# Windowed attention and two MLPs on one core: the first steps reordered, a gate in its own buffers, and an addition moved between engines

## The reference

```python
# q, k, v: (4, 8, 576, 64) float32; window 64
scores = (1/sqrt(64)) * q @ k.T                       # per batch and head
rel = pos[:, None] - pos[None, :]
scores = where((rel >= 0) & (rel < 64), scores, -1e9)
scores = scores - max(scores)
attn = exp(scores); attn = attn / (sum(attn) + 1e-09)
x = (attn @ v) as (2304 tokens, 512)
# first MLP: d_model 512, d_ff 1536
xn = x / sqrt(mean(x*x) + 1e-06) * rms_g
g = xn @ w_gate
x = (g * sigmoid(g) * (xn @ w_val)) @ w_out
# second MLP: d_ff 2048
h = x @ w_in
out = (h * sigmoid(1.702 * h)) @ w_out2
```

## Time and profile before

| | us |
|---|---|
| median of 3 runs | 904.75 |
| lowest and highest | 903.81 and 905.58 |
| the profiled execution, whole | 904.1 |
| its span, first to last instruction | 901.6 |
| TensorE busy, in the span | 889.1 |
| VectorE busy | 539.6 |
| ScalarE busy | 398.5 |
| POOL busy | 82.2 |
| mean granted TensorE clock | 0.998 of 2.4 GHz |

### The profile page before, as it was taken

The page is one execution under the profiler, slowest core; times in us unless marked ns, Lnnn a source line. Parts: engine busy times, 40 slices in busy tenths (PEclk is TensorE's granted clock), DMA queues, the critical chain, the costliest instruction groups (busy, mean ns, idle before and its releaser), DMA issues.

```text
span 901.6 us, 14706 instructions
## 1 busy us (share of the span) xinstructions
PE 889.1 (99%) x5372; PEld 771.3 (86%) x5372; DVE 539.6 (60%) x1256; ACT 398.5 (44%) x941; POOL 82.2 (9%) x114
## 2 busy tenths in 40 slices
PE   8899999999999999999999999999999999999998
PEld 7799888888888888888888899999999999999997
DVE  6886634334333343433336578887788788867663
ACT  5676333343333423334123354545464554545442
POOL 6234001030010300113000000000000000000000
PEclk9999999999999999999999999999999999999999
DMA  7672111102111021100500222121432122241201
GB/s 253 205 218 96 51 51 51 50 24 74 51 50 51 24 73 51 51 25 1 186 1 24 94 96 69 60 81 47 164 117 94 48 74 67 67 145 47 71 24 70
DMA packets 41078, 69.75 MB, mean 77 GB/s; under 512 B 3632, under 2 KB 13872, under 8 KB 41008
## 3 DMA queue, kind: packets, MB, share of 16 engines
q1 hardware_dynamic: 39600, 67.12, 23.0%
q10 hardware_dynamic: 1408, 1.70, 0.6%
HBM read 59.38 MB, written 9.44 MB: 76 GB/s over the span
## 4 chain that ended last, share of the span: by engine, by line
PE 94%; DVE 3%; ACT 2%; issue 1%; POOL 1%; POOLq 0%; ACTq 0%; DVEq 0%
PE ps L631 16%; PE ps L633 15%; PE ps L632 15%; PE ps L825 7%; PE ps L826 7%; PE ps L824 7%; PE ps L767 7%; PE ps L763 7%; PE ps L765 6%; PE ps L612 2%; PE ps L584 2%; PE ps L598 2%; DVE w_all L1197 1%; ACT prob L867 0%; DVE sig L1235 0%
## 5 line engine op out<-in xcount | busy, mean ns | idle before, releaser
L631 PE MATMUL ps<-x_hi,w_all 128*128 128x512 f32 (+1 forms) x480 | 179.4, 374 | 0.2 <-DVE x_lo L1137 0.2
L633 PE MATMUL ps<-x_lo,w_all 128*128 128x512 f32 (+1 forms) x480 | 176.7, 368 | 0.0
L632 PE MATMUL ps<-x_hi,w_all 128*128 128x512 f32 (+1 forms) x480 | 176.7, 368 | 0.0
L826 PE MATMUL ps<-w2out,hB 128*128 128x512 f32 x288 | 113.0, 392 | 0.0
L825 PE MATMUL ps<-w2out,hB 128*128 128x512 f32 x288 | 112.9, 392 | 0.0
L824 PE MATMUL ps<-w2out,hB 128*128 128x512 f32 x288 | 112.0, 389 | 0.0
L631 PEld LDWEIGHTS ps<-x_hi,w_all 128*128 128x128 f32 x480 | 90.4, 188 | 18.4 <-issue 3.0
L633 PEld LDWEIGHTS ps<-x_lo,w_all 128*128 128x128 f32 x480 | 90.4, 188 | 15.3
L632 PEld LDWEIGHTS ps<-x_hi,w_all 128*128 128x128 f32 x480 | 90.4, 188 | 14.6
L1235 DVE SCALAR_TENSOR_TENSOR sig<-sig,ps 128x512 f32<-128x512 f32 x48 | 32.9, 686 | 107.1 <-ACT sig L981 107.1
L631 PE MATMUL ps<-h_hi,w_all 128*128 128x512 f32 (+1 forms) x240 | 90.4, 376 | 1.8 <-DVE hid L1244 1.6
(11 more groups left out here) (144 smaller groups left out, 1557.0 us busy)
## 6 DMA issues: line engine op xcount, KB each, us to landing
wstage<-in_w_b SPq DMA_DIRECT2D x48, 512.0 KB, 3.7
wstage<-in_w_a SPq DMA_DIRECT2D x36, 256.0 KB, 3.2
vwin<-in_v_win SPq DMA_DIRECT2D x32, 256.0 KB, 3.9
kwin<-in_k_t SPq DMA_DIRECT2D x32, 160.0 KB, 3.3
x2raw<-x_scratch SPq DMA_DIRECT2D x3, 1536.0 KB, 7.5
out_dram<-yB SPq DMA_DIRECT2D x18, 256.0 KB, 4.4
qtok<-in_q_t SPq DMA_DIRECT2D x34, 128.0 KB, 2.6
x_scratch<-wstage SPq DMA_DIRECT2D x3, 1024.0 KB, 4.2
```

What stands on the lines that cost most here:

```text
L631: pe.matmul(out_, w[:, 0, cols], xh, start=first, stop=False, **flags)
L632: pe.matmul(out_, w[:, 1, cols], xh, start=False, stop=False, **flags)
L633: return pe.matmul(out_, w[:, 0, cols], xl, start=False, stop=last, **flags)
L826: ins = pe.matmul(y, hB_of(g, chunk, 1)[:, rows], w[:, 0, chunk, :], start=False, stop=last)
```

## The change

It has three parts. (1) In the first four steps the orders on all four engines are changed: the transposes of a step go ahead of the product with V of the step before, two groups of fillers go, ScalarE takes four of the first nine casts where it had one, in which (0, 1) is between the copies and (2, 1) behind `inverse_rms(0)`, and VectorE's splits follow a new order `FIRST_SPLITS`. That order also sets the numbers that SP's loads wait for. (2) In tile 0 the scaled gate of chunk 1 lies in `ss` and its tanh in `sq`, so that scaling and tanh of chunk 1 run directly behind those of chunk 0. (3) From step 4 on the 1e-9 is added to the sums by ScalarE, in an activation of 128x4 with a wait for its own exponentials, and VectorE makes only the reciprocal. Besides, the splits (4, 0) and (4, 1) of tile 0 stand behind the normalising of step 5, where (4, 0) was between those of steps 4 and 5.

```diff
+        def scaled_of(c):
+            return ss[:, GT:2 * GT] if c == 1 else gsc
+
+        def silu_of(t, c):
+            return sq[:, :] if (t, c) == (0, 1) else sig[:, 0:TILES_A[t][1]]
...
+        FIRST_SPLITS = ((0, 0), (0, 1), (1, 0), (1, 1), (2, 0), (0, 2), (2, 1), (1, 2), (2, 2))
+
         def splitsA(c, m):
-            return 3 * c + m + 1
+            return FIRST_SPLITS.index((c, m)) + 1 if c < 3 else 3 * c + m + 1
+
+        CASTS_BY_ACT = ((0, 1), (1, 1), (2, 0), (2, 1)) + tuple((c, m) for c in range(3, CA) for m in range(2))
+        CASTS_BY_POOL = ((0, 0), (1, 0), (0, 2), (1, 2)) + tuple((c, 2) for c in range(2, CA))
...
@@ gpsimd
             weights_hi_A(0, 0)
             normalise(1)
             normalise(2)
-            weights_hi_A(0, 1)
             normalise(3)
-            weights_hi_A(0, 2)
             weights_hi_A(1, 0)
             add_early_square(1)
-            weights_hi_A(1, 1)
-            weights_hi_A(1, 2)
+            weights_hi_A(0, 2)
             add_early_square(2)
             add_early_square(3)
-            weights_hi_A(2, 1)
+            weights_hi_A(1, 2)
             weights_hi_A(2, 2)
...
@@ tensor
             keep_busy(3, 2)
+            transpose_probs(2)
             probs_by_v(1)
-            transpose_probs(2)
+            transpose_probs(3)
             pe.wait_ge(max_ready, EARLY)
-            keep_busy(4, 2)
             probs_by_v(2)
-            transpose_probs(3)
-            first_chunk_part(0)
             probs_by_v(3)
-            for d in range(1, DC):
+            for d in range(DC):
                 first_chunk_part(d)
...
@@ scalar
                 ins.then_inc(exp_done, 1)
+                if s >= EARLY:
+                    act.wait_ge(exp_done, s + 1)
+                    act.wait_ge(consts_ready, 2)
+                    by = rsum[:, s % EARLY, :]
+                    nc.scalar.activation(by, by, ACT.Identity, bias=guard[:, 0:1]).then_inc(sums_guarded, 1)
...
             first_x_hi(0)
+            weights_hi_by_act(0, 1)
+            copy_probT(2)
             first_x_hi(1)
-            copy_probT(2)
-            first_square(0)
             copy_probT(3)
-            first_square(1)
             first_x_hi(2)
-            first_square(2)
             first_x_hi(3)
+            for s in range(EARLY):
+                first_square(s)
+            weights_hi_by_act(1, 1)
             nc.scalar.preload_act_table_set(LN_SET)
-            first_square(3)
             weights_hi_by_act(2, 0)
             act.wait_ge(consts_ready, 1)
             inverse_rms(0)
+            weights_hi_by_act(2, 1)
...
-                    tanh_A(t, c)
+                    if (t, c) != (0, 1):
+                        tanh_A(t, c)
+                    if (t, c) == (0, 0):
+                        tanh_A(0, 1)
...
@@ vector
             def reciprocal_of_sum(s):
+                if s >= EARLY:
+                    dve.wait_ge(sums_guarded, s - EARLY + 1)
+                    wait(dve, probs_normed, s - EARLY + 1)
+                    nc.vector.reciprocal(rrec[:, s % EARLY, :], rsum[:, s % EARLY, :]).then_inc(late_rec, 1)
+                    return
...
             weights_lo_A(0, 0)
+            reciprocal_of_sum(3)
             evacuate_probT(1)
-            reciprocal_of_sum(3)
             dve.wait_ge(g_loaded, 16)
             first_x_lo(0)
             weights_lo_A(0, 1)
             first_x_lo(1)
-            weights_lo_A(0, 2)
+            weights_lo_A(1, 0)
             first_x_lo(2)
-            weights_lo_A(1, 0)
             first_x_lo(3)
             weights_lo_A(1, 1)
+            weights_lo_A(2, 0)
+            weights_lo_A(0, 2)
+            weights_lo_A(2, 1)
             weights_lo_A(1, 2)
-            weights_lo_A(2, 0)
-            weights_lo_A(2, 1)
...
-                    if t == 0:
+                    if t == 0 and c != 1:
                         scale_gate(c)
+                    if t == 0 and c == 0:
+                        scale_gate(1)
                     if scored is not None:
                         reciprocal_of_sum(scored)
                         normalise(scored)
-                    if split is not None and c > 0:
+                    if split is not None and c > 0 and c != 2:
                         weights_lo_A(split, 0)
...
                         normalise(scored + 1)
+                    if split is not None and c == 2:
+                        weights_lo_A(split, 0)
                     if split is not None and c > 0:
                         weights_lo_A(split, 1)
```

More of the change, by code:

```diff
@@ L79, in fused_attention_mlps @@
         eps = sb("eps", [P, 1], F32)
+        guard = sb("guard", [P, 1], F32)
         with ExitStack() as at:
@@ L202, in fused_attention_mlps @@
         rec_order = sem("rec_order")
+        late_rec = sem("late_rec")
+        sums_guarded = sem("sums_guarded")
         probs_normed = sem("probs_normed")
         probs_transposed = sem("probs_transposed")
+        first_probT_ready = sem("first_probT_ready")
         probT_ready = sem("probT_ready")
@@ L255, in wait, with wait_probT @@
                 eng.wait_ge(s, value)
+        def wait_probT(eng, n):
+            if n <= 2:
+                wait(eng, first_probT_ready, n)
+            else:
+                eng.wait_ge(probT_ready, n - 2)
         def slotA(c):
@@ L261, in raw @@
             return wstage[:, (3 * u + m) * DM:(3 * u + m + 1) * DM]
+        FIRST_SPLITS = ((0, 0), (0, 1), (1, 0), (1, 1), (2, 0), (0, 2), (2, 1), (1, 2), (2, 2))
         def splitsA(c, m):
-            return 3 * c + m + 1
+            return FIRST_SPLITS.index((c, m)) + 1 if c < 3 else 3 * c + m + 1
+        CASTS_BY_ACT = ((0, 1), (1, 1), (2, 0), (2, 1)) + tuple((c, m) for c in range(3, CA) for m in range(2))
+        CASTS_BY_POOL = ((0, 0), (1, 0), (0, 2), (1, 2)) + tuple((c, 2) for c in range(2, CA))
         def cast_by_act(c, m):
-            return (c, m) == (2, 0) or (c > 2 and m < 2)
+            return (c, m) in CASTS_BY_ACT
         def casts_so_far(by_act, c, m):
-            return sum(cast_by_act(*at_) == by_act for at_ in itertools.product(range(CA), range(3)) if at_ <= (c, m))
+            return (CASTS_BY_ACT if by_act else CASTS_BY_POOL).index((c, m)) + 1
         A11, A12, A22, S1, S2, S3, S4 = range(COMBOS)
@@ L497, in _ @@
             nc.gpsimd.memset(eps[:, :], 1.0e-6).then_inc(consts_ready, 1)
+            nc.gpsimd.memset(guard[:, :], 1.0e-9).then_inc(consts_ready, 1)
             def normalise(s):
@@ L576, in scores @@
                 elif s % 2 == 0:
-                    pe.wait_ge(probT_ready, s)
+                    wait_probT(pe, s)
                     pe.wait_ge(ln_done, home_of(s)[0])
@@ L591, in transpose_probs @@
                 if s < EARLY:
-                    wait(pe, probT_ready, s - 1)
+                    wait_probT(pe, s - 1)
                 else:
@@ L606, in probs_by_v @@
                 pe.wait_ge(v_loaded[slot(s)], 16 * uses(s))
-                pe.wait_ge(probT_ready, s + 1)
+                wait_probT(pe, s + 1)
                 for m in range(GB // 2):
@@ L620, in sum_squares @@
                     pe.wait_ge(early_sums, EARLY - 1)
-                    pe.wait_ge(probT_ready, EARLY - 1)
+                    wait_probT(pe, EARLY - 1)
                     pe.matmul(ps[:, ATT_BANK, 0:n], ones[:, :], ss[:, 0:n], start=True,
@@ L662, in gate @@
                     pe.wait_ge(x_lo_ready, 2)
-                    pe.wait_ge(probT_ready, EARLY)
+                    wait_probT(pe, EARLY)
                 elif t == 0 and c == 2:
@@ L979, in tanh_A @@
                     act.wait_ge(gate_done, n + 1)
-                wait(act, hidA_made, n)
-                nc.scalar.activation(sig[:, 0:w], gsc[:, :] if t == 0 else gate_of(t, c),
+                wait(act, hidA_made, n if (t, c) != (0, 1) else 0)
+                nc.scalar.activation(silu_of(t, c), scaled_of(c) if t == 0 else gate_of(t, c),
                                      ACT.Tanh, scale=0.5).then_inc(sigA_ready, 1)
@@ L1126, in normalise @@
             def normalise(s):
-                dve.wait_ge(rec_order, 2 * s + 2)
+                dve.wait_ge(late_rec, s - EARLY + 1)
                 by = rrec[:, s % EARLY, :].rearrange("p (d n o) -> p d n o", d=2, o=1).to_broadcast([P, 2, GB // 2, P])
@@ L1132, in evacuate_probT @@
                 dve.wait_ge(probs_transposed, s + 1)
-                nc.vector.tensor_copy(probT_of(s), pt_of(s)).then_inc(probT_ready, 1)
+                nc.vector.tensor_copy(probT_of(s), pt_of(s)).then_inc(first_probT_ready, 1)
             def first_x_lo(s):
@@ L1229, in scale_gate @@
                 dve.wait_ge(rinv_ready, 1)
[L1230 removed]
+                nc.vector.tensor_tensor(scaled_of(c), gate_of(0, c), rinv0[:, :], ALU.mult).then_inc(gate_scaled, 1)
             def silu_A(t, c):
@@ L1234, in silu_A @@
                 dve.wait_ge(sigA_ready, n + 1)
-                nc.vector.scalar_tensor_tensor(out=sig[:, 0:w], in0=sig[:, 0:w], scalar=1.0,
```

(5 more changed lines are left out.)

## The result

The changed kernel takes 907.76 us (median of 8 runs, 906.87 to 908.63) against 904.40 us for the kernel before (8 runs beside them): a ratio of 1.0036, 95% interval 1.0025 to 1.0047. It is slower by 3.4 us, more than the 0.2% that tell a change from none here. The profiled execution took 907.83 us, its span 905.6 us. The time lies in the range of the prediction, above its point of 905.9; the change went the way of rival B.

What follows compares the result with a forecast made beforehand. Only the first 45 us, through row_max(4) and its distance to row_max(6), could move the end; -1.1, +2.9, -0.9, +0.7, +0.1 and -0.65 gave +1.05, rounded to +1.1: median 905.9 us, range 904.0 to 908.5.

Steps and rivals of the forecast that it cites:

- rival B: Slower, 906.7 to 909: the weights' burst lands slowly (+2.4), or TensorE falls to 1.2 GHz uncovered (+2.8); chance 0.36.
- R: Start of row_max(4) on VectorE, 31.00 us before; forecast 32.6, +1.6, bounds +0.5 and +3.0.
- Steps 0 to 3: TensorE's reordered start: sum of squares at 20.75 instead of 21.87, 1.1 us earlier, bounds 0.6 and 1.5.
- VectorE's first splits: Two splits ahead of scale_gate(0) wait for ScalarE's casts: scale_gate(0) at 25.7 instead of 23.86, 1.8 us later.
- SP's queue: Load (2,2) waits for the sixth split, delaying q, k, v and chunk 3's weights; late scores hidden, the burst not.
- +0.7 for weights that land late: Sum's term for chunk 3's weights landing late in the burst, taking R from 31.9 to 32.6.
- A: The forecast case: the loss at scale_gate(0) eats what the new buffers win, 905.9, spanning 904.7 to 906.6; chance 0.47.
- Own buffers: Chunk 1's scale_gate(1) fills the wait for the first tanh, -0.9 us; removing TensorE's 1.6 us wait is worth nothing itself.
- The guard: ScalarE's addition to the sums: 0.3 us each, hidden later, costing up to 0.8 us in all if cover is gone.
- rival D: The guard's function isn't in the loaded set; each brings two 1.28 us table loads, 915 or more; chance 0.02.
- the same distances as before: Behind row_max(6), the later landmarks were to follow at unchanged distances.
- Rival C: Faster, 902.3 likely: TensorE's early waits vanish as shorter splits bring VectorE early to scale_gate(0); chance 0.15.

Runs made afterwards that it cites:

- a3: The changed kernel with cast (2,1) made by POOL, behind (1,2), in place of ScalarE; 907.04 us, 1.0036 of the kernel before.
- b1: The changed kernel with cast and split (0,2) moved early and cast (2,1) made by POOL; 903.60 us, 0.9995 of the kernel before.
- b2: The kernel before with only chunk 1's scaled gate and tanh in buffers of their own; 903.43 us, ratio 0.9996.
- a4: The changed kernel with 1e-9 added by VectorE in all steps, no guard on ScalarE; 907.53 us, 1.0043 of the kernel before.
- b5: The kernel before with own buffers and split (4,0) moved behind normalise(5), without the guard on ScalarE; 903.53 us, ratio 0.9999.
- b6: The kernel before with own buffers, guard on ScalarE and split (4,0) moved, first steps in the old order; 903.12 us, ratio 0.9993.
- d1: b1 with ScalarE's copies of the transposed probabilities ahead of the same chunk's tanh in tile 0; 902.53 us, 0.9989 of the kernel before.
- d2: d1 without the guard on ScalarE; 902.62 us, 0.9986 of the kernel before.
- c1: The changed kernel with q, k, v of steps 4 and 5 ahead of load (2,2), load (3,0) held late; 905.52 us, 1.0016 of the kernel before.
- a2: The changed kernel with cast and split (0,2) moved early, so load (2,2) waits for the fourth split; 904.97 us, 1.0013 of the kernel before.

## Why the prediction was right or wrong

**What bounds the kernel** held. Nothing moved behind 100 us, and R with the way from it to row_max(6) set the end: R shifted by +3.85 and row_max(6) by +3.33, and "end = R's shift - 0.5" gave the second from the first within 0.1. That the ratio's +3.3 is the same number is in part luck: the two profiled executions differ by 4.06 at the sum of squares and by 4.0 in their spans.

**Steps 0 to 3**: the sum of squares, predicted 1.1 earlier, is at 21.05 instead of 21.87: 0.8 earlier. **VectorE's first splits**: scale_gate(0), predicted at 25.7, +1.8, is at 25.94, +2.1, behind the wait for cast (2,1) (24.08 to 24.7) that was named. By itself this step is hidden in the changed kernel (a3) and worth 1.7 us once the loads are in time (b1).

**SP's queue**: the mechanism was right in each link (q at 22.96, predicted 22.5; w(3,0) at 25.82, predicted 25.3; scores at 27.08, predicted 25.9, covered). The term that was mis-sized is "+0.7 for weights that land late". 5.41 us went by between issue and landing, and VectorE's wait for it was 2.68. With it R = 25.94 + 6.2 + 2.7 = 34.8, against 34.85 measured: 1.05 above the top of my bounds, 33.8. Two steps made it small. I took the 6 us of the old kernel's w(3,2) for an exception, with "others land in 3.3"; that number is k's, and the weights of the same burst took 6.2 us (w(3,0)) and 6.3 us there. And I counted from w(3,2), with 1.6 us behind it, where the load that binds is w(3,0), with 3.6 us of cast and VectorE's queue behind it (31.26 to 34.85); w(3,2) was cast at 32.62 and split at 34.24, without a wait of VectorE. My own issue time, 25.3, with 6.2 and 3.6 would have given 35.1.

The range held the result because it took in most of rival B. A, which I put first, ended at 906.6. Rival B, "the burst lands as the slow load of rows 9 did", is what happened. Its other half, a fall of the clock behind 42 us, isn't: TensorE stood for 0.69, 1.52 and 1.40 us between 38.1 and 44.4, about as forecast, and the granted clock was 1.00 from 32 us on. The clock had fallen from 28.5 to 31.9 us, under cover (window of 1 us, the last column but two is the granted clock):

```profile
28.00:29.00 1.00, 0.86 (x17) 0.53 (x17) 0.80 (x2) 0.16 (x1) 0.00 (x0) 0.73 1.02 275
29.00:30.00 1.00, 1.00 (x7) 1.00 (x6) 0.22 (x1) 0.00 (x0) 0.00 (x0) 0.50 1.03 285
...
42.00:43.00 1.00, 1.00 (x9) 0.84 (x7) 1.00 (x4) 0.00 (x0) 0.00 (x0) 1.00 0.40 41
```

**Own buffers**: "worth nothing by itself" held (b2). The 0.9 us for the covered tanh is in the changed kernel, where R - scale_gate(0) without the wait is 6.2, but not in b2, and most of it isn't the buffers' doing. In the kernel before, the first tanh starts at 24.91, when the table load is over, 1.05 us behind scale_gate(0); in the changed kernel scale_gate(0) comes 2.1 us later and the tanh only 0.45 us behind it, at 26.39. scale_gate(1) fills 0.34 us of the wait, and the delay of scale_gate(0) took the rest. The number was right for a reason that I didn't give.

**The guard** took 0.30 us on ScalarE, the value chosen, and moved nothing. The Trainium skill's figure for such an activation ("ScalarE: Activation LUTs", What ACT_TABLE_LOAD costs, about 0.28 us) agrees with this row. No table was loaded around it, so rival D is out; this agrees with the Trainium skill, "ScalarE: Activation LUTs", The hidden batching unit, that identity is in every set.

**The moved split** and **the copies**: R+5.36 and R+8.11 against R+5.4 and R+8.15; -0.52 to row_max(6) against -0.55.

**Behind row_max(6)** I forecast "the same distances as before", with up to 0.8 if the cover failed. From row_max(6) to the sum of squares it is 40.55 in place of 39.82: 0.7 lost, in two waits for copies of 0.6 and 0.36 us. Without the guard (a4) it is 40.29. But a3 and b1, which have the changed kernel's code there, show 39.81 and 39.83, and b5 and b6 40.36 and 39.83: the distance differs between executions by as much as it does between kernels, so no cause of the 0.7 is shown. In d1 and d2, with the copies ahead of the tanh, it is 39.61 and 39.39, the shortest two; there the waits for copies are gone.

**Rival C** fell: VectorE's splits did get shorter (0.65 to 0.83 us for six of the eight, 1.07 on average before), and it helped nothing, since VectorE waited 1.1, 1.1 and 2.2 us for ScalarE's casts between them.

## What to carry to other kernels

When the order of work is changed on one engine, read every queue that counts that engine's completions: the number is a position, and a load that waits for "the third split" waits for another piece of work once the order is new. What stands behind a blocked transfer in its queue is as late as it is, needed or not, and it leaves in one burst. Here a late issue without the burst cost nothing at R (c1), and the burst without the late issue nothing either (the kernel before, 6.2 us for the same load); both together cost 2.7 us of VectorE's time. When a landing time is taken from a row, it should be that of the same load in the same company. A long wait in the list of waits isn't its own price: in a2 and in c1 TensorE's stop of 3.9 us for k vanished and came back as one of 3.4 and 3.5 us at the next place where it asked for VectorE's work.

## What the runs showed of the hardware that I had not expected

How long a transfer of 256 KB takes depends on what is issued around it. Behind 1.1 MB of q, k and v issued in the 3 us before it, w(3,0) took 5.4 us from issue to landing in the changed kernel and 6.2 us in the kernel before; with nearly the same issue time and q, k and v moved away (c1) it took 2.5 us. In the 5 us from 22 to 27 us the core's DMA engines were busy for 0.60 of the time in the changed kernel and for 0.27 in c1. And TensorE, after standing still for 3.9 us, still began at full clock and fell to 1.2 GHz only at 28.5 us, 1.4 us after it had resumed work, for 3.4 us.
